# Seven products of blocks in place of eight: the second layer's two factors by Strassen's scheme

## The reference, cut to what matters

```python
attn = retention(q, k, v)                  # 4 x 8 heads, 576 tokens, 64 wide
x = attn as (2304 tokens, 512)
h = x @ w_in                               # 512 -> 2048
g = where(h >= 1, h, where(h <= -1, 0, (h + 1)**2 / 4))
x = g @ w_out                              # 2048 -> 512
a = x @ w_a;  b = x @ w_b                  # 512 -> 1536 each, the two factors
out = (a * b) @ w_out2                     # 1536 -> 512
```

## Time and profile before

| | us |
|---|---|
| median of 3 runs | 913.02 (912.96 to 913.7) |
| the profiled execution | 915.21 |
| its span, first to last instruction | 912.7 |
| TensorE busy | 902.3 (99% of the span), 5160 matmuls |
| VectorE busy | 348.2 (38%) |
| ScalarE busy | 285.0 (31%) |
| DMA | 42.46 MB, mean 47 GB/s |

### The profile page before, as it was taken

The page is one execution under the profiler, slowest core; times in us unless marked ns, Lnnn a source line. Parts: engine busy times, 40 slices in busy tenths (PEclk is TensorE's granted clock), DMA queues, the critical chain, the costliest instruction groups (busy, mean ns, idle before and its releaser), DMA issues.

```text
span 912.7 us, 12087 instructions
## 1 busy us (share of the span) xinstructions
PE 902.3 (99%) x5160; PEld 766.0 (84%) x5160; DVE 348.2 (38%) x565; ACT 285.0 (31%) x476; POOL 36.7 (4%) x54
## 2 busy tenths in 40 slices
PE   7999999999999999999999999999999999999998
PEld 6998888888899888888888888888899888888886
DVE  4686655434445433546653213111222311131112
ACT  1245454333445333535542112111211211121111
POOL 4550000000000000000000000000000000000000
PEclk9999999999999999999999999999999999999999
DMA  9996000000000000013330000100010000010001
GB/s 344 313 357 236 1 0 1 1 1 1 1 1 1 1 1 1 1 69 105 104 104 1 0 1 10 38 1 0 1 47 2 24 0 1 1 47 0 1 1 46
DMA packets 20053, 42.46 MB, mean 47 GB/s; under 512 B 1568, under 2 KB 12320, under 8 KB 20000
## 3 DMA queue, kind: packets, MB, share of 16 engines
q1 hardware_dynamic: 19856, 41.50, 13.1%
q10 hardware_dynamic: 144, 0.20, 0.1%
HBM read 36.97 MB, written 4.72 MB: 46 GB/s over the span
## 4 chain that ended last, share of the span: by engine, by line
PE 98%; DMA 1%; DVE 0%; ACT 0%; POOL 0%; issue 0%; SPq 0%; POOLq 0%
PE score_b L386 5%; PE score_a L386 5%; PE score_b L385 5%; PE score_a L385 5%; PE score_a L384 5%; PE score_b L384 5%; PE score_a L332 4%; PE kv_b L349 4%; PE score_a L333 4%; PE kv_b L350 4%; PE score_b L333 4%; PE score_a L334 4%; PE ret_b L350 4%; PE score_b L332 4%; PE ret_b L349 4%; PE ret_b L351 4%
## 5 line engine op out<-in xcount | busy, mean ns | idle before, releaser
L501 DVE TENSOR_TENSOR gate_w<-relu_s,relu_r 128x512 f32<-128x512 f32 (+1 forms) x80 | 51.1, 639 | 131.6 <-ACT relu_r L613 131.6
L385 PE MATMUL score_b<-xl,w_all 128*128 128x512 f32 (+1 forms) x240 | 88.3, 368 | 0.0
L386 PE MATMUL score_b<-xh,w_all 128*128 128x512 f32 (+1 forms) x240 | 88.3, 368 | 0.0
L385 PE MATMUL score_a<-xl,w_all 128*128 128x512 f32 (+1 forms) x240 | 88.3, 368 | 0.0
L386 PE MATMUL score_a<-xh,w_all 128*128 128x512 f32 (+1 forms) x240 | 88.3, 368 | 0.0
L384 PE MATMUL score_a<-xh,w_all 128*128 128x512 f32 (+1 forms) x240 | 88.2, 368 | 0.0
L384 PE MATMUL score_b<-xh,w_all 128*128 128x512 f32 (+1 forms) x240 | 88.2, 368 | 0.0
L622 ACT ACTIVATE gh<-gated 128x512 fp32r<-128x512 f32 (+1 forms) x80 | 47.2, 590 | 105.0 <-DVE gated L504 105.0
L530 DVE TENSOR_TENSOR gated<-score_a,relu_s 128x512 f32<-128x512 f32 (+1 forms) x30 | 19.1, 638 | 156.9 <-ACT relu_s L642 156.9
L510 DVE TENSOR_TENSOR gl<-gated,gh 128x512 fp32r<-128x512 f32 (+1 forms) x80 | 51.1, 638 | 50.8 <-ACT gh L622 50.6
L530 DVE TENSOR_TENSOR gated<-score_b,relu_s 128x512 f32<-128x512 f32 (+1 forms) x30 | 19.1, 637 | 126.6 <-ACT relu_s L642 126.6
(11 more groups left out here) (107 smaller groups left out, 1930.4 us busy)
## 6 DMA issues: line engine op xcount, KB each, us to landing
kq<-k_q SPq DMA_DIRECT2D x16, 576.0 KB, 6.4
w_raw<-w SPq DMA_DIRECT2D x12, 768.0 KB, 4.2
kvt<-kv_tok SPq DMA_DIRECT2D x16, 512.0 KB, 5.7
w1a_raw<-w SPq DMA_DIRECT2D x10, 512.0 KB, 9.8
out<-x_all SPq DMA_DIRECT2D x18, 256.0 KB, 3.0
w1b_raw<-w SPq DMA_DIRECT2D x6, 512.0 KB, 5.8
decays<-decays_c SPq DMA_DIRECT2D x3, 193.5 KB, 6.7
vtail<-v_tail SPq DMA_DIRECT2D x16, 32.0 KB, 5.5
```

The costliest lines, as they stand in the source:

```text
L385: pe.matmul(o, w2_slab(f, 0)[:, at], xl[:, k, 0:WIDTHS[t]], start=False, stop=False)
L386: mm = pe.matmul(o, w2_slab(f, 1)[:, at], xh[:, k, 0:WIDTHS[t]], start=False, stop=(k == KT - 1))
L501: nc.vector.tensor_tensor(gate_w[:, 0:WIDTHS[t]], relu_s[:, 0:WIDTHS[t]], relu_r[:, 0:WIDTHS[t]], ALU.add).then_inc(gatew_ready, 1)
```

## The change

Layer two alone is rewritten; layer one gets the preparation of weights beside it. What it does:

- **Seven products.** Tokens go in three tiles (`NS`) of 768, each in two halves of 384 (`HALF`). Input features are two blocks of 256, the two factors are two block columns: a 2 x 2 by 2 x 2 product of blocks, with seven block products (Strassen's scheme in Winograd's form) in place of eight. One block product for one block f of hidden features is 2 x 3 matmuls of 384 columns. Sums of blocks of x (`difference`) and of weights (`block_sums`) are made by VectorE. A step u is one tile and one f: 36 steps.
- **Sums in PSUM and SBUF.** Products 1, 6, 7 and 4 are added one after another in a bank of the step (`main_b`, two of them), 5 and 3 in another, 2 in a third. ScalarE copies U1 (product 1), product 5 and U2 (1 + 6) to SBUF; VectorE adds these to the banks for `a0`, `b1`, `a1`, multiplies (`prod1`, `prod0`), and the products are rounded and split as before, in halves of 384 (`ph`, `pl`).
- **Weight operands made once, kept in DRAM.** For each f the seven 256-wide operands, high and low, are made during layer one at 12 given steps (`prep_steps`), two stores to `w2_ops` in DRAM (0.92 MB each). In layer two every step loads its 1.835 MB from there into one of three buffers (`wop`, `WBUF`).
- **Outputs by groups.** Four blocks f are a group (`GROUP`). For each 128 tokens a share of a group is 12 matmuls of 512 columns into one bank, in two halves; then ScalarE copies the bank to `x_all` (first group of a tile) or VectorE adds it (other two). Shares begin five steps (`LAG`) behind, three half-shares in each step. The output weights are loaded group by group (`load_out`, 1.049 MB into one of two buffers) and rounded and split again for each tile.

The core of the diff, the new SP queue and TensorE's order (the old functions `products`, `outputs`, `load_w2`, `copy_out` go):

```diff
+HALF = 384
+SUPER = 2 * HALF
+ROWS = SUPER // P
+XBUF = 8
+WBUF = 3
+GBUF = 8
+GROUP = 4
+LAG = 5
+            def load_ops(u):
+                if u < WBUF:
+                    end = XBUF * 2 * SUPER + 2 * WOP * (u + 1)
+                    sp.wait_ge(y_done, NF1 * (NT - 1) + (end - 1) // (2 * W1) + 1)
+                else:
+                    sp.wait_ge(p4_done, u - WBUF + 1)
+                sp.wait_ge(op_stored, 32 * (u % NF2 + 1))
+                sp.dma_start(raw(wop[u % WBUF][:, :, :]), w2_ops[u % NF2]).then_inc(wop_loaded[u % WBUF], 16)
+            def load_out(q):
+                if q < 2:
+                    sp.wait_ge(h_ready, NF1 * NT)
+                    sp.wait_ge(y_done, NF1 * NT)
+                else:
+                    sp.wait_ge(rows_done, ROWS * (q - 1))
+                at = (q * GROUP) % NF2
+                sp.dma_start(wo_raw[q % 2][:, :, :],
+                             w2_out[at:at + GROUP].rearrange("f p c -> p f c")).then_inc(wo_loaded[q % 2], 16)
...
+            for u in range(WBUF):
+                load_ops(u)
+            load_out(0)
+            load_out(1)
...
+            for u in range(WBUF, STEPS2):
+                load_ops(u)
+                if u % GROUP == 0 and u >= 2 * GROUP:
+                    load_out(u // GROUP)
+                if u % NF2 == NF2 - 1 and u > NF2:
+                    store_rows(u // NF2 - 1)
+            store_rows(NS - 1)
...
+        def slots(step):
+            if step < STEPS2 + 1:
+                mine = range(3 * (step - LAG), 3 * (step - LAG) + 3)
+                return [(v // 2, v % 2) for v in mine if v >= 0]
...
+            def rows(n, half):
+                q, a = n // ROWS, n % ROWS
+                last = GROUP * q + 2 * half + 1
+                pe.wait_ge(pl_ready, 2 * last + 2)
+                pe.wait_ge(wo_ready, last + 1)
...
+                if half == 1:
+                    mm.then_inc(rows_done, 1)
+            def step2(u):                      # TensorE
+                mine = slots(u)
+                if u < STEPS2:
...
+                        pe.wait_ge(prod0_ready, u - 1)
+                    pe.wait_ge(wop_loaded[u % WBUF], 16 * (u // WBUF + 1))
+                    product(1, u, main_b[u % 2], True).then_inc(p1_done, 1)
...
+                        pe.wait_ge(a0_ready, u)
+                    product(2, u, p2_b, True).then_inc(p2_done, 1)
...
+                    pe.wait_ge(u2_copied, u)
+                    product(7, u - 1, main_b[(u - 1) % 2], False).then_inc(p7_done, 1)
+                for n, half in mine[0:1]:
+                    rows(n, half)
+                if u < STEPS2:
...
+                        pe.wait_ge(a1_ready, u)
+                    product(5, u, p5_b, True).then_inc(p5_done, 1)
+                if u:
+                    pe.wait_ge(b1_ready, u)
+                    product(4, u - 1, main_b[(u - 1) % 2], False).then_inc(p4_done, 1)
+                for n, half in mine[1:2]:
+                    rows(n, half)
+                if u < STEPS2:
+                    pe.wait_ge(u1_copied, u + 1)
+                    product(6, u, main_b[u % 2], False).then_inc(p6_done, 1)
+                    pe.wait_ge(p5_copied, u + 1)
+                    product(3, u, p5_b, False).then_inc(p3_done, 1)
+                for n, half in mine[2:3]:
+                    rows(n, half)
```

```diff
+            load_ab(0)
+            for f in range(NF2):
+                if f + 1 < NF2:
+                    load_ab(f + 1)
+                store_ops(f)
```

More of the change, by code:

```diff
@@ L42, with build @@
 CONST = MASKS + P + 2 + 1
[L45 to L55, removed]
+W_AT = {1: 0, 2: 1, 4: 2, 5: 3, 6: 4, 7: 5, 3: 6}
+X_AT = {1: 0, 2: 1, 5: 2, 6: 3, 3: 4, 7: 5, 4: 6}
+def build(nc, k_q, kv_tok, v_tail, w1, w2_ab, w2_out, decays_c, out):
     ctx = ExitStack()
@@ L146, in build @@
         y_copied = sem("y_copied")
[L147 to L150, removed]
+        p1_done = sem("p1_done")
+        p2_done = sem("p2_done")
+        p7_done = sem("p7_done")
+        p5_done = sem("p5_done")
+        p4_done = sem("p4_done")
+        p6_done = sem("p6_done")
+        p3_done = sem("p3_done")
+        u1_copied = sem("u1_copied")
+        u2_copied = sem("u2_copied")
+        a0_ready = sem("a0_ready")
+        p5_copied = sem("p5_copied")
+        a1_ready = sem("a1_ready")
+        b1_ready = sem("b1_ready")
+        prod1_ready = sem("prod1_ready")
+        prod0_ready = sem("prod0_ready")
+        ph1_ready = sem("ph1_ready")
+        ph0_ready = sem("ph0_ready")
         pl_ready = sem("pl_ready")
-        o_done = sem("o_done")
-        o_copied = [sem(f"o_copied{a}") for a in range(TT)]
+        rows_done = sem("rows_done")
+        rows_out = [sem(f"rows_out{i}") for i in range(4)]
         o_stored = sem("o_stored")
@@ L160, in w1_raw @@
             return w1_raws[f][:, :]
[L162 to L166, removed]
         def raw(ap):
@@ L368, in _ @@
             project(NT - 1, NF1 - 2)
[L370 to L375, removed]
-                else:
[L377 to L425, removed]
+            def product(p, u, o, start):
+                j = u // NF2
+                if u % NF2 == 0:
+                    pe.wait_ge(xop_ready, OPS * j + X_AT[p] + 1)
+                w, b = wop[u % WBUF], x_buffer(j, X_AT[p])
+                for k in range(2):
+                    at = slice(W_AT[p] * AW + k * P, W_AT[p] * AW + (k + 1) * P)
+                    pe.matmul(o, w[:, 0, at], xop_hi[b][:, k, :], start=(start and k == 0), stop=False,
+                              skip_group_check=True)
+                    pe.matmul(o, w[:, 0, at], xop_lo[b][:, k, :], start=False, stop=False,
+                              skip_group_check=True)
+                    mm = pe.matmul(o, w[:, 1, at], xop_hi[b][:, k, :], start=False, stop=(k == 1),
+                                   skip_group_check=True)
+                return mm
@@ new lines, in rows @@
+            def rows(n, half):
+                q, a = n // ROWS, n % ROWS
+                last = GROUP * q + 2 * half + 1
+                pe.wait_ge(pl_ready, 2 * last + 2)
+                pe.wait_ge(wo_ready, last + 1)
+                if n < 4:
+                    pe.wait_ge(y_copied, KT * NT)
+                elif half == 0:
+                    pe.wait_ge(rows_out[n % 4], n // 4)
+                o = y_b[n % 4]
+                for u in (last - 1, last):
+                    hi = ph[u % GBUF][:, a * P:(a + 1) * P]
+                    lo = pl[u % GBUF][:, a * P:(a + 1) * P]
+                    w_hi, w_lo = wo_hi[q % 2][:, u % GROUP, :], wo_lo[q % 2][:, u % GROUP, :]
+                    pe.matmul(o, hi, w_hi, start=(u % GROUP == 0), stop=False)
+                    pe.matmul(o, hi, w_lo, start=False, stop=False)
+                    mm = pe.matmul(o, lo, w_hi, start=False, stop=(u % GROUP == GROUP - 1))
+                if half == 1:
+                    mm.then_inc(rows_done, 1)
@@ L427, in _ @@
+            for u in range(STEPS2 + 1):
+                step2(u)
+            for n, half in slots(STEPS2 + 1):
+                rows(n, half)
         @block.vector
@@ new lines, in split_out, with add_rows @@
+            def split_out(u):
+                dve.wait_ge(wo_hi_ready, u + 1)
+                at = (u // GROUP) % 2
+                nc.vector.tensor_tensor(wo_lo[at][:, u % GROUP, :], wo_raw[at][:, u % GROUP, :],
+                                        raw(wo_hi[at][:, u % GROUP, :]), ALU.subtract).then_inc(wo_ready, 1)
+            def add_rows(step, place):
+                for n in shares_ended(step, place):
+                    if not first_share(n):
+                        dve.wait_ge(rows_done, n + 1)
+                        nc.vector.tensor_tensor(o_rows(n), y_b[n % 4].rearrange("p (k i) -> p k i", k=KT),
+                                                o_rows(n), ALU.add).then_inc(rows_out[n % 4], 1)
@@ L519, in _ @@
                         split_w1(f + EARLY)
[L520 to L534, removed]
@@ L556, in _ @@
+            for u in range(STEPS2 + 1):
+                step2(u)
+            add_rows(STEPS2, 2)
+            for place in range(2 * ROWS):
+                add_rows(STEPS2 + 1, place)
         @block.scalar
@@ L670, in constants @@
+            for u in range(STEPS2 + 1):
+                step2(u)
+            copy_rows(STEPS2, 2)
 def constants():
```

391 lines of the change are left out of this document (292 added, 99 removed).

## The result

The changed kernel takes 968.58 us (median of 4 runs, 967.85 to 970.22) against 913.13 us, the median of four runs of the kernel before: ratio 1.061, 95% interval 1.059 to 1.063. It was forecast at 970 (950 to 988), slower. The profiled execution has a span of 966.9 us.

A forecast was written before the change was run, and what follows sets the result against it. TensorE was taken as the bound, busy 902.3 of 912.7 us. Profiled 915.2 - 33.8 + 1.5 + 2.0 - 0.3 + 71.4 + 16.1 = 972.1 us; the median, 2.2 lower, gave 969.9, said as 970, range 950 to 988.

The forecast's parts named there:

- Part 1: Layer two on TensorE: 1512 product matmuls of 384 columns, 261.8 for 295.6 us, output matmuls unchanged; gain 33.8 us.
- Part 2: VectorE and ScalarE in layer two: no bound, only small waits for b1 and product 5's copy; together 1.5 us.
- Part 3: Layer one: making weight operands delays low halves in the 256-token tile about 1 us each; 2 us, between 0 and 4.
- Part 4: SP's queue in layer two: operand loads behind a group's wait stop TensorE seven times, 10.2 us each, 71 us.
- Part 5: TensorE's clock in layer two: half rate after each stop, 2.3 us each, seven 16 us.
- (a): Rival on TensorE in layer two: the stops are there but the clock stays high; 954 us, 8%.
- (b): Rival on layer two's stops: covered, given at least 10 us, about one step, of cover; 883 us, faster, 6%.
- (c): Rival on SP's queue: three transfers issued together share the engines, 4.3 us more a stop; 1000 us, 6%.
- (d): Rival on layer two's products: weight loads bound the shorter matmuls, 188 instead of 173 ns, 23 us more; 993 us, 2%.

The follow-up runs named there:

- experiment 3: The changed kernel with the wait in the same place of SP's queue, but the operands issued before the output weights: 946.69 us.
- experiment 5: The changed kernel with 50 more matmuls of 384 columns on TensorE ahead of product 1 in steps 9, 13, ... 33: 955.41 us.
- cover_8us: As order_swapped, but the operand load of steps 9, 13, ... 33 also waits for product 7 of the step before, 8.2 us ahead of use: 882.90 us.
- before_tiles_of_384: The kernel before with six tiles of 384 tokens in place of 512, 512, 256, 512, 512: 926.12 us, ratio 1.014.
- experiment 6: The run of before_tiles_of_384: the kernel before with its widths changed to six tiles of 384 tokens; 926.12 us, ratio 1.014.
- order_swapped: The changed kernel with SP issuing the operand load of step 4q+1 before the wait for output-weight group q: 882.46 us, ratio to before 0.966.

## Why the prediction was right, point by point

- **Part 1, products: -33.8 forecast.** 1512 x 0.1735 = 262.3 for 295.6 us: -33.3. The midpoint was good to 0.2%. What it missed are the output matmuls: the prediction kept them at 226.7 ns, they take 231, and 648 x 0.004 = +2.6 us.
- **Part 2, other engines: +1.5 forecast.** One wait of 0.4 us on ScalarE's copy of product 5, in step 1 as named (0.6 forecast); the wait for `b1` in the first step of a tile did not come. Over-sized by 1.1. The row, of the weight loads' waits:

```profile
PEld score_b L518 <- ACT p L952: 0.4, 1, 0.4
```

- **Part 3, layer one: +2.0 forecast, 0.0 measured.** The term failed, though the total hides it. I had two low halves of the 256-token tile about 1 us late each and took that for a wait of TensorE. They are late by about as much, and TensorE does not wait for them. An ordinary low half in that tile and its first use two steps later, then the late one behind the first preparation and its use:

```profile
265.06 0.42 DVE L725 TENSOR_TENSOR gl<-gated,gh 128x256 fp32r<-128x256 f32 x1 [0.49 <-ACT gh L902]
```

```profile
257.74 0.43 DVE L725 TENSOR_TENSOR gl<-gated,gh 128x256 fp32r<-128x256 f32 x1 [0.48 <-ACT gh L902]
...
259.74 0.28 PE L489 MATMUL kv_b<-gh,w1a 128*128 128x256 f32 x1
```

  The ordinary one ends at 265.48 us and is used from 268.38 on, 2.9 us later, since TensorE runs two steps ahead. The late one ends at 258.17 and is used from 259.74 on, 1.6 us later; the one behind the second preparation (275.71, used at 277.01) has 1.3 us left. So 1.3 to 1.6 us of lateness were there, and 2.9 us of slack took them in, which the estimate had left out.
- **Part 4, the stops: 71.4 forecast, 71.4 measured**, at the steps named. That the total is exact is luck in part: the second transfer's share was under-sized (2.5 against 2.9 us) and the lone load's over-sized (7.7 with the semaphore, against 7.3). The Trainium skill's page DMA: Bandwidth & Descriptors (Specifications) gives some 358 GB/s for one core from HBM. As a limit the trace disagrees with it also in the stops, with 433 GB/s from 550 to 553 us; as the mean price of the 1.05 MB of experiment 3 it is met. The 8 us more that the stops would have taken by it did not come.
- **Part 5, the clock: 16.1 forecast, 14.7 measured** (86.1 - 71.4), of which about 2 are there with the clock kept too (0.3 us a stop in experiment 5). Experiment 5 shows the mechanism. This is as the section "HAM oscillation — how this bites in real kernels" of the Trainium skill's TensorE: Matmul & The Clock Gate says of DMA waits that come back; here it is seven times of seven for stops of 10.2 us. That the size came so near is luck in part: 2.3 us a stop was the middle of a range from 0 to 4.5.
- **Sum.** 970 against 968.6. The errors of -2.0 (layer one), -1.1 (small waits), -1.4 (clock), +0.5 (products) and +2.6 (outputs) come to -1.4, so errors of 7.6 us in all cancel for the most part.
- **Rivals.** (a), no clock loss, fell: 0.50 granted. (b), the stops covered, was not what the kernel does, but its number, 883, is what the kernel takes once they are (882.5). The 10 us of cover that it asks for hold for this kernel, where both transfers stand behind the wait; with the operands first 7.2 are enough, and cover_8us has no stop with 8.2. (c) fell with experiment 3, (d) with 0.1735 us a matmul.

## What to carry to other kernels

Read a hand-ordered DMA queue like an engine: for each wait in it, look up who needs the transfer issued next, and whether the event waited for is earlier than that need by more than a landing. Two lines in the wrong order turned a gain of 3.4% into a loss of 6.1%, and the busy times say only that TensorE has gaps (884.5 us, 91%), not why; the row of TensorE's waits for the DMA, the row of SP's own waits and the clock row do. A stop of TensorE costs more than its idle time, so stops of a few us that recur are worth removing before anything is made faster.

## What the runs showed of the hardware that was not expected

- Stops of only 2.4 us already lowered the granted clock to 0.50 in some places (three of seven) and not in others of equal length, and in two of the three only some 1 us after TensorE had resumed. Stops of 4.8, 7.3 and 10.2 us lowered it each time, and cost about the same beyond their idle time: 2.2, 1.9 and 2.1 us, so in these runs the price went by the number of stops and not by their length.
- Matmuls of 512 columns start 0.227 us apart in long runs of their kind, and 0.231 us apart in groups of 6 or 9 between matmuls of 384 columns, each of them and not only the first. It is not the traffic: before_tiles_of_384 moves nothing between 600 and 610 us, where the 0.231 of experiment 6 was read. The cause is open.
- 439 GB/s into SBUF beside dense matmuls (order_swapped, 550 to 553 us) cost TensorE nothing that shows: its matmuls of 384 columns start 0.1734 us apart from 547 to 557 us and 0.1736 us apart over the whole of 540 to 830 us.
